# Three rearrangements in a fused attention and gated-MLP kernel: where the value means are summed, when x is copied, when the fused weights are multiplied

## The chip, the cores and the metric

The kernel runs on one core of a Trainium2 chip. The metric is the device time of one execution in microseconds (us), as the median of three runs. TensorE (PE) does matmuls and transposes into PSUM, which has eight banks of 512 fp32 columns; ScalarE (ACT), VectorE (DVE) and GpSimd (POOL) do the rest, and the SyncE queue (SP) issues all DMAs. The program is written with explicit semaphores: each engine has its own list of instructions in order, and a wait holds back everything behind it on that engine.

## The reference

Inputs are q, k, v (2 batches, 8 heads, 768 positions, 64 per head), `w_val`, `w_out` (512 x 512), 5 taps of convolution weights for 512 channels, `w_in` (512 x 1024), `w_spatial` (768 x 768), `b_spatial` and a last `w_out2`.

```
k_sum = k.reshape(B, H, nb, 32, D).max(axis=3)
v_sum = v.reshape(B, H, nb, 32, D).mean(axis=3)
scores = [q k^T / 8 where |i-j| < 16, else -1e9 ; q k_sum^T / 8 + log(32)]
x = softmax(scores) @ [v ; v_sum]                      # (B, S, 512)
gate = sigmoid(causal 5-tap convolution of x per channel)
y = (gate * (x @ w_val)) @ w_out
h = relu(y @ w_in); u, v = halves of h; v normalised over its 512 channels
out = (u * (w_spatial @ v + b)) @ w_out2
```

## The kernel before

Heads are handled in pairs: PAIRS = 8 pairs, T = 6 steps of 128 query positions for each, STEPS = 48 steps `i`, with `p, t = divmod(i, T)`. For each group of 64 queries the local keys (96) and the 24 block maxima stand side by side in `k_win` (120 columns); the local values and the 24 block means stand in `v_win`.

The loops over steps are software-pipelined by hand. In step i PE does: the scores of step i (L613), one turn (transpose) of a piece of k (t = 0, 1, 2) or q (t = 3, 4, 5) of the next pair (L578), in step 6p+2 the means of pair p (L654, six matmuls of `v_nat` with a selection matrix), the transposes of the probabilities of step i-5 (`turn_probs`, L627) and the values of step i-6 (L642). DVE masks the scores and takes their maximum (L976), normalises (L996), copies turned k (L1003) and the second head's turned q (L1014), and takes block maxima (L1029). ACT does: the copy of the turned probabilities of step i-5 (`take_probsT`, L847), in step 6p+2 the copy of the means (`take_means`, L863), the copy of the first head's turned q (L821), the exponentials of step i (L833, one for each head, each followed by a read of its accumulator), and in even steps the copies of two steps of x (L853 the first head, L856 the second; one in three of the latter is DVE's). POOL spreads the means into `v_win` (L507), then completes `k_win` of the next pair (`k_tails`, L471 to L475), splits x into two fp32r halves (L512, L526) and adds pairs of v rows ahead of the means (L495).

PSUM: banks 0 and 1 hold scores, bank 2 the turned probabilities in columns 0 to 255 and the means in 256 to 383, bank 3 reciprocals, banks 4 and 5 alternate for the turned pieces of k and q (`bank_qk(n)` is bank 4 + n % 2, columns 0 to 255, n = 0, 1, 2 for k and 3, 4, 5 for q) and later of w_out, banks 6 and 7 hold x. As the means share bank 2 with the turned probabilities, PE has ahead of the means a wait for the copy of the last probabilities, and ahead of the `turn_probs` after them one for the copy of the means (`clear_probs`).

After the steps comes a second part: 16 `val` groups (x w_val by channel block and half a batch, 12 matmuls each), 8 `fused` groups (w_out w_in, 12 matmuls each), the convolution on DVE (8 instructions for each of 8 channel blocks, L1050, after a first tap on ACT, L875, in banks 4 and 5), the gate (tanh on ACT, L887), gate times val (`work`, L1115) on DVE, its high half on ACT (L923) and low half on POOL (L526), and for fused groups a high half on ACT (L926) and a low half on DVE (L1120). The groups rotate through six banks in the order of the list `groups`: a group waits until the one six places ahead of it in the list has been taken. The lists `groups` and `between` put fused group j behind val group FUSED_AFTER[j]; ACT, DVE and POOL follow `between`. The first two val groups are computed in the last steps of attention. Then follow u, v, spatial and output groups on PE (L697 too).

## Time and profile before

| | us |
|---|---|
| median of 3 runs | 308.68 (308.52 to 309.01) |
| the profiled execution's own time | 308.57 |
| its span, first to last instruction | 306.8 |
| PE busy, PE weight loads busy | 293.8 (96%), 268.6 (88%) |
| DVE, ACT, POOL busy | 173.9, 150.9, 123.4 |

A matmul's end is modelled, so PE's busy time is not work at its peak, and a recorded end may lie behind the start of the next instruction. A wait is shown on the engine that waits, with the instruction that ended it. Times in the rows are counted from the start of the span.

### The profile page before, as it was taken

What the parts mean: (1) busy time and instruction counts of PE and PEld (TensorE: products, weight loads), DVE (VectorE), ACT (ScalarE), POOL (GpSimd) and SP (SyncE); (2) the same over time, 40 slices, a digit from 0 to 9 for tenths busy, and PEclk for the clock granted to TensorE, in tenths of its full rate; (3) what the DMA queues carried; (4) which work ended last, traced back from release to release, by engine and by line L of the source; (5) the groups of instructions that cost most, each with busy time, mean ns of one, the idle gap of its engine ahead of it and who ended that gap; (6) DMA issues with size and microseconds to landing.
All of it is one profiled execution on the core that took longest, in us unless ns stands there. A gap on an engine that the chain in (4) does not pass through costs nothing.

```text
span 306.8 us, 5354 instructions
## 1 busy us (share of the span) xinstructions
PE 293.8 (96%) x1768; PEld 268.6 (88%) x1768; DVE 173.9 (57%) x578; ACT 150.9 (49%) x464; POOL 123.4 (40%) x140
## 2 busy tenths in 40 slices
PE   7789999999999999989999999999999999999996
PEld 6788888988889899887999998888899999988885
DVE  5899888998788867778300006787755242310000
ACT  3689999999997764442422234433332111122221
POOL 6434887777534884223300001343476323220000
DMA  7999999984610633000000001121010000002222
GB/s 160 213 207 233 228 194 185 252 225 117 168 49 0 189 88 103 0 2 0 1 2 0 0 2 51 51 80 41 35 34 2 0 0 2 0 35 90 83 103 103
DMA packets 51801, 25.52 MB, mean 83 GB/s; under 512 B 44586, under 2 KB 46910, under 8 KB 51774
## 3 DMA queue, kind: packets, MB, share of 16 engines
q1 hardware_dynamic: 51774, 25.18, 33.6%
q8 instruction: 14, 0.23, 0.3%
q14 instruction: 13, 0.11, 0.1%
HBM read 22.03 MB, written 3.15 MB: 82 GB/s over the span
## 4 chain that ended last, share of the span: by engine, by line
PE 63%; ACT 20%; issue 7%; DVE 6%; POOL 2%; DMA 1%; ACTq 0%; DVEq 0%; POOLq 0%
PE psum L697 54%; ACT probs L833 7%; DVE psum L1050 4%; ACT probsT L847 2%; ACT qT L821 2%; PE psum L654 2%; ACT xT L856 2%; ACT psum L875 2%; PE psum L673 1%; PE psum L613 1%; PE psum L578 1%; ACT xT L853 1%; PE psum L785 1%; PE psum L627 1%; DVE gate L1050 1%
## 5 line engine op out<-in xcount | busy, mean ns | idle before, releaser
L526 POOL TENSOR_TENSOR g_lo<-work,g_hi 128x384 fp32r<-128x384 f32 x32 | 32.3, 1024 | 46.9 <-ACT g_hi L957 26.2
L526 POOL TENSOR_TENSOR vn_lo<-work,vn_hi 128x512 fp32r<-128x512 f32 x12 | 15.5, 1293 | 61.3 <-DVE vn_hi L1152 61.3
L833 ACT ACTIVATE probs<-neg_s,neg_max 128x120 f32<-128x120 f32 x96 | 37.0, 392 | 0.7 <-DVE neg_max L976 0.5
L642 PE MATMUL psum<-probsT,v_win 120*128 120x128 f32 x192 | 29.9, 278 | 0.0
L613 PE MATMUL psum<-k_win,qT 128*128 128x120 f32 x192 | 29.0, 274 | 0.8 <-DVE qT L1014 0.7
L976 DVE CUSTOM_DVE_ANT_0 neg_s<-psum,mask 128x120 f32<-128x120 f32 x96 | 24.6, 277 | 5.2 <-PE psum L613 4.8
L1050 DVE SCALAR_TENSOR_TENSOR psum<-xT,conv_c,psum 128x384 f32<-128x384 f32 x48 | 26.0, 616 | 1.2 <-ACT psum L875 1.0
L613 PEld LDWEIGHTS psum<-k_win,qT 128*128 128x128 f32 x192 | 25.2, 191 | 1.2 <-issue 0.9
L642 PEld LDWEIGHTS psum<-probsT,v_win 120*128 120x128 f32 x192 | 25.2, 191 | 0.8 <-issue 0.2
L1130 DVE TENSOR_TENSOR wsp_lo<-psum,wsp_hi 128x384 fp32r<-128x384 f32 x12 | 6.6, 549 | 33.3 <-ACT wsp_hi L938 33.3
L957 ACT ACTIVATE g_hi<-work 128x384 fp32r<-128x384 f32 x16 | 8.3, 523 | 34.6 <-DVE work L1164 34.6
L1162 DVE TENSOR_TENSOR work<-psum,b_row 128x384 f32<-128x384 f32 x16 | 8.9, 558 | 28.2 <-PE psum L697 26.6
L627 PE MATMUL psum<-ident,probs 128*120 128x128 f32 x96 | 19.1, 281 | 3.5 <-ACT probsT L847 3.0
L847 ACT ACTIVATE probsT<-psum 120x256 f32<-120x256 f32 x48 | 18.2, 379 | 5.1 <-PE psum L627 4.8
L931 ACT ACTIVATE u<-psum 128x384 f32<-128x384 f32 x16 | 7.9, 491 | 25.8 <-PE psum L697 25.8
L996 DVE TENSOR_TENSOR probs<-probs,psum 128x240 f32<-128x240 f32 x48 | 19.1, 400 | 1.0
L964 ACT ACTIVATE work<-psum 128x512 f32<-128x512 f32 (+1 forms) x13 | 7.3, 565 | 24.8 <-PE psum L697 23.7
L697 PE MATMUL psum<-wsp_lo,vn_hi 128*128 128x384 f32 x96 | 19.4, 336 | 0.0
L697 PE MATMUL psum<-wsp_hi,vn_lo 128*128 128x384 f32 x96 | 19.4, 336 | 0.0
L697 PE MATMUL psum<-wsp_hi,vn_hi 128*128 128x384 f32 x96 | 19.3, 335 | 0.0
L833 ACT ACTIVATION_READ_ACCUMULATOR probs<-neg_s,neg_max 128x1 f32 x96 | 18.9, 197 | 0.0
L627 PEld LDWEIGHTS psum<-ident,probs 128*120 128x120 f32 x96 | 11.1, 137 | 7.0 <-ACT probsT L847 6.2
(125 smaller groups left out, 721.1 us busy)
## 6 DMA issues: line engine op xcount, KB each, us to landing
v_win<-in_v_dram SPq DMA_DIRECT2D x16, 240.0 KB, 3.3
k_nat<-in_k_dram SPq DMA_DIRECT2D x16, 192.0 KB, 5.0
v_nat<-in_v_dram SPq DMA_DIRECT2D x8, 384.0 KB, 3.9
out_dram<-work SPq DMA_DIRECT2D x11, 256.0 KB, 2.0
q_nat<-in_q_dram SPq DMA_DIRECT2D x14, 192.0 KB, 4.4
raw<-in_moe_w_spatial_dram SPq DMA_DIRECT2D x6, 384.0 KB, 3.1
raw<-in_moe_w_out_dram SPq DMA_DIRECT2D x8, 256.0 KB, 2.8
raw<-in_moe_w_in_dram SPq DMA_DIRECT2D x8, 256.0 KB, 2.8
```

The lines of the kernel that those rows point to most:

```text
L526: nc.gpsimd.tensor_tensor(dst_lo, src, dst_hi.bitcast(F32), ALU.subtract).then_inc(lo_sem, 1)
L613: ins = nc.tensor.matmul(bank_s(i)[:, g, :], qT[:, s, 2 * t + g, :], k_win[:, s, 2 * t + g, :], start=True, stop=True)
L627: ins = nc.tensor.transpose(bank_t[:, g, :], probs[:, i % RING, g, :], ident[:, :])
L642: ins = nc.tensor.matmul(bank_x(i)[:, i % 2 * 2 + g, :], v_win[0:KEYS, s, 2 * t + g, :], probsT[0:KEYS, i % 2, g, :], start=True, stop=True)
L697: ins = nc.tensor.matmul(o, lhs[a][c], rhs[b][c], start=(part == 0 and c == 0), stop=(part == 2 and c == n - 1))
L833: ins = nc.scalar.activation(probs[:, i % RING, g, :], neg_s[:, i % 3, g, :], ACT.Exp, bias=neg_max[:, i % 4, g:g + 1], scale=-1.0, accum_ ...
L847: nc.scalar.activation(probsT[0:KEYS, i % 2, :, :], bank_t, ACT.Copy).then_inc(probsT_ready, 1)
L957: nc.scalar.activation(g_hi[:, c, w], work[:, g % 3, 0:HALF], ACT.Copy).then_inc(g2_hi_ready, 1)
L976: nc.vector.tensor_tensor_reduce(out=neg_s[:, i % 3, g, :], in0=bank_s(i)[:, g, :], in1=mask[:, e, :], scale=-(float(D) ** -0.5), scalar=B ...
L996: nc.vector.tensor_tensor(a, a, r, ALU.mult).then_inc(probs_ready, 1)
L1050: nc.vector.scalar_tensor_tensor(out=o, in0=x, scalar=w, in1=acc, op0=ALU.mult, op1=ALU.add).then_inc(conv_step, 1)
L1162: nc.vector.tensor_tensor(y, bank("spatial", g, HALF), b_row[:, w], ALU.add).then_inc(b_added, 1)
```

## The change

The means go from bank 2 to columns 256 to 383 of bank 4, and on PE from the middle of step 6p+2 to the end of steps 3, 7, 13, 19, 25, 31, 37 and 44, behind the values; ACT copies them at the beginning of the step after. The waits follow the bank: the wait for the means' copy stands ahead of `turn_k(p, 2)` from pair 2 on, of `turn_q(1, 1)` and of the later w_out turns, and no longer ahead of `turn_probs`; the means wait for the copy of the piece that was in bank 4. The second head's copy of x on ACT goes from even steps to the odd step behind. FUSED_AFTER is two larger throughout, and DVE does the next channel block's taps ahead of its part of a fused group.

```diff
--- before.py
+++ after.py
@@ -220,7 +220,7 @@
         def by_group(x):
             return x.rearrange("p (g n) -> p g n", n=GROUP)
 
-        bank_m = psum[:, 2, 2 * P:3 * P]
+        bank_m = psum[:, 4, PIECE:PIECE + P]
 
         def bank_s(i):
             return psum[:, i % 2, 0:2 * KEYS].rearrange("p (g n) -> p g n", n=KEYS)
@@ -335,6 +335,8 @@
         between += [("fused", n) for n in range(len(FUSED_AFTER), 2 * C)]
 
         LATER = 2 * (TAPS - 1)
+
+        means_at = [T // 2] + [T * p + 1 for p in range(1, PAIRS - 1)] + [STEPS - T + 2]
 
         def channels(g):
 
@@ -586,12 +588,16 @@
                     pe.wait_ge(qB_ready, PIECES * (p - 1) + 2 + piece)
                 elif piece == 2:
                     pe.wait_ge(kT_ready, PIECES * p + 1)
+                    if p >= 2:
+                        pe.wait_ge(v_mean_ready, p)
                 turn(k_nat, p, piece, k_loaded, k_turned)
 
             def turn_q(p, piece):
 
                 if piece < 2:
                     pe.wait_ge(kT_ready, PIECES * p + 2 + piece)
+                    if p == 1 and piece == 1:
+                        pe.wait_ge(v_mean_ready, 1)
                 else:
                     pe.wait_ge(qA_ready, PIECES * p + 1)
                     pe.wait_ge(qB_ready, PIECES * p + 1)
@@ -614,15 +620,10 @@
                                            start=True, stop=True)
                 ins.then_inc(scores_ready, 1)
 
-            def clear_probs(i):
-
+            def turn_probs(i):
+                pe.wait_ge(probs_ready, i + 1)
                 if i >= 1:
                     pe.wait_ge(probsT_ready, i)
-                if (i + 2) % T == 0 and i + 2 < STEPS:
-                    pe.wait_ge(v_mean_ready, (i + 2) // T + 1)
-
-            def turn_probs(i):
-                pe.wait_ge(probs_ready, i + 1)
                 for g in range(2):
                     ins = nc.tensor.transpose(bank_t[:, g, :], probs[:, i % RING, g, :], ident[:, :])
                 ins.then_inc(probs_turned, 1)
@@ -648,8 +649,11 @@
                 pe.wait_ge(v_nat_added, p + 1)
                 if p == 0:
                     pe.wait_ge(sel_step, 4)
+                    pe.wait_ge(kT_ready, 2 * PIECES)
+                elif p < PAIRS - 1:
+                    pe.wait_ge(kT_ready, PIECES * (p + 1) + 1)
                 else:
-                    pe.wait_ge(v_mean_ready, p)
+                    pe.wait_ge(wout_split, 1)
                 for j in range(RUN // 2):
                     ins = nc.tensor.matmul(bank_m[0:KEYS], sel[:, j, :], v_nat[:, p % 2, :, 2 * j * D:(2 * j + 1) * D],
                                            start=(j == 0), stop=(j == RUN // 2 - 1))
@@ -659,6 +663,7 @@
                 wait_piece(pe, W_OUT + c)
                 if c >= 2:
                     pe.wait_ge(wout_split, c - 1)
+                    pe.wait_ge(v_mean_ready, PAIRS)
                 else:
                     pe.wait_ge(qA_ready, PIECES * (PAIRS - 1) + 2 + c)
                     pe.wait_ge(qB_ready, PIECES * (PAIRS - 1) + 2 + c)
@@ -748,13 +753,11 @@
                     n, term = divmod(i - STEPS, 3)
                     val(n, (term,))
                 if 5 <= i < STEPS + 5:
-                    clear_probs(i - 5)
-                if p < PAIRS and t == 2:
-                    means(p)
-                if 5 <= i < STEPS + 5:
                     turn_probs(i - 5)
                 if 6 <= i:
                     values(i - 6)
+                if i in means_at:
+                    means(means_at.index(i))
 
             for kind, n in groups[VALS_IN:place["u", 0]]:
                 if kind == "val":
@@ -846,15 +849,18 @@
                     act.wait_ge(x_summed, i - 1)
                 nc.scalar.activation(probsT[0:KEYS, i % 2, :, :], bank_t, ACT.Copy).then_inc(probsT_ready, 1)
 
-            def take_x(j):
+            def take_xA(j):
 
                 act.wait_ge(x_summed, 2 * j + 2)
                 p, r = divmod(2 * j, T)
                 nc.scalar.activation(by_group(x_of(p, r * P, 2 * P)[0:D]), bank_x(2 * j)[0:D, :, 0:GROUP],
                                      ACT.Copy).then_inc(xA_ready, 1)
-                if not x_on_dve(j):
-                    nc.scalar.activation(by_group(x_of(p, r * P, 2 * P)[D:P]), bank_x(2 * j)[D:P, :, GROUP:P],
-                                         ACT.Copy).then_inc(xB_ready, 1)
+
+            def take_xB(j):
+
+                p, r = divmod(2 * j, T)
+                nc.scalar.activation(by_group(x_of(p, r * P, 2 * P)[D:P]), bank_x(2 * j)[D:P, :, GROUP:P],
+                                     ACT.Copy).then_inc(xB_ready, 1)
 
             def take_means(p):
                 act.wait_ge(means_summed, p + 1)
@@ -892,18 +898,20 @@
                 turned_q(0, piece)
             act.wait_ge(conv_turned, 1)
             nc.scalar.activation(conv_c[:, :], bank_x(0)[:, 0, 0:TAPS * C], ACT.Copy).then_inc(conv_ready, 1)
-            for i in range(STEPS + 7):
+            for i in range(STEPS + 8):
                 p, t = divmod(i, T)
+                if i - 1 in means_at:
+                    take_means(means_at.index(i - 1))
                 if 5 <= i < STEPS + 5:
                     take_probsT(i - 5)
-                if p < PAIRS and t == 2:
-                    take_means(p)
                 if p + 1 < PAIRS and t >= PIECES:
                     turned_q(p + 1, t - PIECES)
                 if i < STEPS:
                     exponentials(i)
                 if i >= 8 and i % 2 == 0:
-                    take_x((i - 8) // 2)
+                    take_xA((i - 8) // 2)
+                if i >= 9 and i % 2 == 1 and not x_on_dve((i - 9) // 2):
+                    take_xB((i - 9) // 2)
                 if p == PAIRS - 1 and t in WOUT_AT:
                     turned_wout(WOUT_AT.index(t))
                 if i in FIRST_AT:
@@ -1116,6 +1124,10 @@
                                                    in1=bank("val", n, HALF), op0=ALU.add,
                                                    op1=ALU.mult).then_inc(val_used, 1)
                 if kind == "fused":
+                    if n < len(FUSED_AFTER):
+                        while taps < min(LATER * (FUSED_AFTER[n] // 2 + 3), LATER * B * C):
+                            conv(taps)
+                            taps += 1
                     dve.wait_ge(fused_hi_ready, n + 1)
                     nc.vector.scalar_tensor_tensor(out=(wu_lo, wv_lo)[n // C][:, n % C, :],
                                                    in0=bank("fused", n, DM), scalar=0.5,
@@ -1166,7 +1178,7 @@
 
 RING = 6
 VALS_IN = 2
-FUSED_AFTER = (5, 7, 9, 11)
+FUSED_AFTER = (7, 9, 11, 13)
 WVALS_OF = ((), (), (0,), (1,), (2,), (3,), (), ())
 PIECES_OF = ((), (0,), (1,), (2,), (3,), (4, 5), (6,), (7,))
 WOUT_AT = (0, 1, 3, 4)
```

## Rows read from the trace of the kernel before

**Rows 1.** Busy time by stretches, one cycle of attention; columns: engine busy us, instructions, clock, DMA.
```profile
...
39.81:49.78 9.97, 9.49 (x79) 8.62 (x79) 8.89 (x47) 9.33 (x40) 7.88 (x10) 1.00 0.97 208
...
```

**Rows 2.** Waits of PE over the whole span: total us, times, longest.
```profile
...
PE psum L627 <- ACT probsT L847: 3.0, 8, 0.4
...
PE psum L697 <- DVE work L1115: 1.4, 2, 1.1
...
PE psum L697 <- ACT win_u_hi L841: 0.4, 1, 0.4
...
```

**Rows 3.** Order of time on PE in that cycle: start, us, instructions.
```profile
...
39.81 0.92 PE L654 MATMUL psum<-v_nat,sel 128*120 128x128 f32 x6
40.56 0.38 PE L627 MATMUL psum<-ident,probs 128*120 128x128 f32 x2
...
41.23 0.60 PE L613 MATMUL psum<-k_win,qT 128*128 128x120 f32 x4
...
43.81 0.43 PE L627 MATMUL psum<-ident,probs 128*120 128x128 f32 x2 [0.44 <-ACT probsT L847]
44.08 0.62 PE L642 MATMUL psum<-probsT,v_win 120*128 120x128 f32 x4
...
```

**Rows 4.** Order of time on ACT in that cycle.
```profile
...
40.98 0.38 ACT L847 ACTIVATE probsT<-psum 120x256 f32<-120x256 f32 x1 [0.47 <-PE psum L627]
41.38 0.27 ACT L863 ACTIVATE v_mean<-psum 24x128 f32<-24x128 f32 x1
41.68 0.40 ACT L833 ACTIVATE probs<-neg_s,neg_max 128x120 f32<-128x120 f32 x1
...
42.57 0.38 ACT L853 ACTIVATE xT<-psum 64x256 f32<-64x256 f32 x1
42.97 0.38 ACT L856 ACTIVATE xT<-psum 64x256 f32<-64x256 f32 x1
43.37 0.38 ACT L847 ACTIVATE probsT<-psum 120x256 f32<-120x256 f32 x1
...
45.95 0.37 ACT L853 ACTIVATE xT<-psum 64x256 f32<-64x256 f32 x1
46.22 0.38 ACT L847 ACTIVATE probsT<-psum 120x256 f32<-120x256 f32 x1
...
```

**Rows 5.** Order of time at the start, on ACT, POOL and PE.
```profile
...
12.65 0.27 ACT L863 ACTIVATE v_mean<-psum 24x128 f32<-24x128 f32 x1 [0.84 <-PE psum L654]
...
14.50 0.38 ACT L833 ACTIVATE probs<-neg_s,neg_max 128x120 f32<-128x120 f32 x1
...
12.98 1.46 POOL L507 COPY v_win<-v_mean 24x1536 f32<-24x1536 f32 x1 [1.79 <-ACT v_mean L863]
...
15.06 0.42 POOL L475 COPY k_win<-k_max 128x288 f32<-128x288 f32 x1
...
17.08 0.41 PE L578 MATMUL psum<-ident,k_nat 128*128 128x128 f32 x2 [0.75 <-ACT qT L821]
...
```

**Rows 6.** Order of time on ACT in the last pair.
```profile
...
81.34 0.39 ACT L847 ACTIVATE probsT<-psum 120x256 f32<-120x256 f32 x1
...
83.74 0.38 ACT L847 ACTIVATE probsT<-psum 120x256 f32<-120x256 f32 x1
...
```

**Rows 7.** Order of time on DVE in the second part.
```profile
...
106.77 3.24 DVE L1050 SCALAR_TENSOR_TENSOR psum<-xT,conv_c,psum 128x384 f32<-128x384 f32 x6
...
110.97 1.01 DVE L1115 SCALAR_TENSOR_TENSOR work<-gate,psum 128x384 f32<-128x384 f32 x2
115.03 0.69 DVE L1120 SCALAR_TENSOR_TENSOR wu_lo<-psum,wu_hi 128x512 fp32r<-128x512 f32 x1 [3.05 <-ACT wu_hi L926]
...
```

**Rows 8.** Order of time on PE in the second part.
```profile
...
110.94 1.10 PE L697 MATMUL psum<-win_u_hi,woutT_hi 128*128 128x512 f32 x4
...
113.74 0.86 PE L697 MATMUL psum<-x_hi,wval_hi 128*128 128x384 f32 x4
...
117.91 1.09 PE L697 MATMUL psum<-win_u_hi,woutT_hi 128*128 128x512 f32 x4
...
```

## The prediction

> **What bounds the kernel now.** I read the waits of TensorE first, then the busy time by stretches, then the order of time on each engine. The kernel has three parts: attention (0 to about 96 us, a repeating cycle of six steps for a pair of heads), the val and fused groups mixed with the convolution (about 96 to 138), and TensorE work that runs without a gap to the end. So only what moves the start of the third part moves the time. TensorE's granted clock is 1.00 (the 2.4 GHz level) in the stretch shown and plays no part.
>
> In attention the cycle is 9.97 us long: PE's weight loads fill 8.62 of it, DVE 8.89, ACT 9.33 [rows 1]. ACT is the engine to follow. It has one real gap in a cycle, 0.47 us before the copy of the turned probabilities (`take_probsT`), where it waits for PE [rows 4]. PE at that time is doing the six means matmuls (39.81 to 40.56) and only then the transposes that ACT waits for [rows 3]. This is the stall that the first part of the change is about.
>
> In the second part PE waits 0.4 us once for the high half of w_in and 1.4 us in two pieces (the longer 1.1) for DVE's `work` [rows 2]. Bank recycling is the reason: group g needs the bank of group g-6. DVE is late because it sits in order behind the copy of the fused group: it is idle 3.05 us before it [rows 7]; the next channel's taps, which need nothing of it, are queued behind.
>
> **Part 1, the means.** Call S the moment at which ACT finishes step 6p+1. Today, S to the exponentials of step 6p+2 is 1.28 us. The probabilities' copy starts at 40.98 and the first exponential at 41.68, 0.70 apart, with v_mean between them [rows 4]. The 0.47 of idle, and some 0.1 by which the last exponential before it outlasts its slot, make the rest (an estimate: 0.58).
>
> After: the means run on PE in the previous step, and that does free ACT from waiting for them. But they now lie in bank 4, and the next user of bank 4 is `turn_k(p+1, 2)`, in step 6p+2. It gets a wait for v_mean_ready, and behind it on PE's queue stands `turn_probs`, which ACT's next copy needs. ACT itself takes v_mean immediately before that copy. So ACT hands v_mean to PE and waits for PE to answer:
> - v_mean 0.27 [rows 4];
> - to PE 0.06 (the copy of 43.37 ends at 43.75, PE starts at 43.81) [rows 3, 4];
> - the two transposes of k 0.27 after a wait (43.81 to 44.08) [rows 3];
> - turn_probs 0.38 to its recorded end, and 0.04 to ACT (40.56 plus 0.38, then 40.98) [rows 3, 4].
>
> That is 1.02 us, in which ACT does only v_mean. With 0.27 for the copy (as between 45.95 and 46.22 a copy of like size [rows 4]) the exponentials start at S plus 1.29, against 1.28 today. The stall changes its name and keeps its size, in each of the six cycles with this order. I take zero. Bounds for each cycle: minus 0.2, if the hand-over is quicker for the small v_mean copy; plus 0.2, if PE's later k turn makes DVE late.
>
> The Trainium skill has the rule behind this (PSUM — Partial Sum Buffer, section PSUM bank collisions raise a hardware error): guard by bank and group of 32 partitions, not by address. By it free columns of a bank are no free bank: the wait travels with the means. The waits in the diff follow that rule; no row of before shows the new one.
>
> Two places are not regular cycles.
> - **Start.** v_mean of pair 0 is taken at 12.65 now, two steps before its new place. There it follows the exponentials of step 3, whose last starts at 14.50 [rows 5]. Without the 0.84 idle ahead of v_mean these move up a little, held by DVE's masks, so v_mean comes near 14.5, 1.85 later. POOL's spread of the means (12.98) and, in order behind it, the k tails (last one 15.06 plus 0.42) [rows 5] move by the same, to 17.3. The scores of step 6 wait for these. PE stands idle 0.75 us until 17.08 [rows 5], so that swallows most: scores to 17.85, then turn_k, 0.76 late. At the next means some 0.3 of it comes back, since they no longer stand ahead of the probabilities. Loss 0.45 (0 to 0.8); a step's exponentials and masks can take up the rest.
> - **Last pair.** From 81.34 to 83.74 ACT runs a copy, v_mean, exponentials and both x copies in 2.40 us with no gap, because the w_out copy before it covers the wait [rows 6]. After: copy 0.27, exponentials 0.75, first x copy 0.27, then S to the next copy, 1.02 plus 0.2 for the w_out turn (four transposes instead of two): 2.5. And the second x copy, 0.53 with the slower change-over, falls outside it. Together 0.55 (0.2 to 0.8) lost. PE has work ready from here on, so it reaches the end of attention.
>
> **Part 2, x in alternate steps.** The two copies take 0.40 each start to start (42.57, 42.97, 43.37), a first-head copy alone 0.27 (45.95, 46.22) [rows 4]. The sum is the same wherever the second stands, 0.81. What changes is who waits. `values` of an even step wants both halves; the second is now ready at about S plus 4.2, and PE would like to start at S plus 3.5. ACT's side: from S plus 1.29, two steps of exponentials at 0.75, three copies at 0.27 (x first head, probabilities, q) and the second x copy at 0.5. PE's side: from S plus 0.60, 26 instructions at 0.11 each (four in 0.60 less the tail of 0.17 [rows 3]), 2.9. PE loses 0.7 there, and has it to spare (8.62 of 9.97 [rows 1]); run forward at full rate, its transposes then come within 0.1 of when ACT wants them, three times in a row. I take plus 0.03 a cycle, 0.2 in all (0 to 1.2).
>
> The Trainium skill (ScalarE: Activation LUTs, Rules for kernel authors) budgets about 0.3 us an ACTIVATE plus 0.83 ns an element. For v_mean's 128 elements that is 0.41, where the row has 0.27; eight round trips would be 1.1 us dearer and the sum 309.0. The row stands.
>
> **Part 3, later fused groups and earlier taps.** PE's idle here is 1.8 us [rows 2], and since a recorded end lies 0.17 after the next start (0.92 long, next after 0.75 [rows 3]), three waits cost 2.3 in starts. The fused group two vals later asks for w_in 4.2 us later (two vals, 113.74 to 117.91 [rows 8]), so the first wait is gone. On DVE: the taps of a channel take 4.20 (106.77 to 110.97) [rows 7], two vals 0.93, a fused low half 0.61. DVE was idle 3.05 after 110.97 plus 0.93; now it goes on: taps of channel 4 to 116.1, vals 6 and 7 to 117.0, taps of channel 5 to 121.2, fused 0 to 121.84. Per channel DVE needs 5.8, PE 6.97 (110.94 to 117.91) [rows 8], so after that DVE is ahead for good. One point is tight: fused group 2 takes fused 0's bank. Fused 1 starts at 110.94 now, after two vals and fused 0 (6.97), so these started at 103.97, and without the wait of 0.44 and the 0.17 at about 103.3. From there the six vals 6 to 11 take 12.5 and fused 0 and 1 take 5.6 (2.80 each, 110.94 to 113.74 [rows 8]): PE wants the bank at 121.4 and waits 0.5. All other recycled banks are free over 1 us ahead. Net gain 2.3, less 0.5 less 0.1 for the restart: 1.7 to 2.0; I take 1.9 (0.9 to 2.4). More DVE cover (taps before fused) is free, since those taps have their first tap from ACT one gate before.
>
> **Sum.** Plus 0.45, plus 0.2, plus 0.55, minus 1.9, minus about 0.1 for v_mean standing beside an x copy: minus 0.8. The profiled execution took 308.57 with a span of 306.80; that gives 307.77 and a span of 306.0. The median of before is 0.11 above that execution: 307.9.
>
> **Rivals.**
> - *The means really leave the path.* If PE's wait is met without the round trip, each cycle wins back its 0.6, seven times: 4 us, with part 3 near 303.5 to 305. For it: the gap before the copy is real. Against: ACT's queue has v_mean directly ahead of the copy. Chance 0.08.
> - *Attention eats it all.* Round trip 0.1 dearer in eight places (an exponential is 0.38 to the next, v_mean is priced at 0.27), start and last pair at their upper bounds: 308.1 to 309.2, no change that can be told. Chance 0.30.
> - *PE becomes late in every cycle through the second x copy.* Values waits at S plus 4.2, then scores, masks and exponentials of the following steps shift; it decides from 0.25 us a cycle, when six cycles cost 1.5 more and the sum is plus 0.7: 309.4, slower; at 0.4 it is 310.3. For it: the 0.1 margins. Against: PE's 1.3 us of spare time in the cycle. Chance 0.16.
> - The forecast, 306.9 to 308.0: 0.46.
>
> **How the numbers follow.** A measurement here can tell about 0.2%, 0.6 us: below 308.06 is faster, above 309.3 slower. Faster 0.46 plus 0.08, 0.54; same 0.30; slower 0.16. The range runs from 306.5, the upper bound of part 3 with a start that loses nothing, to 309.4; it leaves out the first rival and the worse half of the third.
>
> **What the profile would show.** ACT's copy L847 still waits some 0.7 us once a cycle, with v_mean just ahead of it; PE's wait at the k turn (L578) is for v_mean; the cycle is 9.9 to 10.1 long; the waits for `work` shrink from 1.4 to about 0.5 and lie near 122; DVE never waits 3 us for wu_hi. Wrong would be: a cycle below 9.7 (the stall was not replaced) or above 10.2 (x copy), or a start of the u groups less than 1.0 earlier against the end of attention.

## The result and the profile after

The change made the kernel slower, by 0.8%: 310.96 us median (310.65 to 311.45, 4 runs) against 308.60 (308.49 to 309.01, 4 runs) for the kernel before, ratio 1.0076 [1.0058, 1.0093]. The prediction said 307.9, range 306.5 to 309.4, faster. The measured time lies above that range. The span of the profiled execution went from 306.8 to 308.9, the clock stayed at 1.00.

The first view is again the busy time of one cycle of attention (from one `v_mean` copy to the next, within 0.02 us; columns as in [rows 1]: PE, PE weight loads, DVE, ACT, POOL).
```profile
51.86:62.14 10.28, 9.03 (x78) 8.66 (x78) 9.31 (x47) 9.22 (x40) 7.87 (x9) 1.00 0.87 199
```
The cycle takes 10.28 us instead of 9.97. ACT's busy time fell, and DVE's rose from 8.89 to 9.31, but DVE has no more work to do: the durations of its 46 instructions add up to 11.9 us in a cycle of either kernel. Busy time counts overlapping records once, and they overlap less where DVE has to wait: a normalisation of 0.40 us is followed by the next mask after 0.32 where nothing waits (46.57 to 46.89 before) and after 0.42 where the mask waits (57.06 to 57.48 in the change). It is waiting that grew. PE's waits (total, times, longest), to be held against [rows 2]:
```profile
PE psum L643 <- ACT xT L862: 5.7, 8, 0.9
PE psum L580 <- ACT v_mean L869: 3.0, 6, 0.7
...
PE psum L619 <- POOL k_win L477: 1.2, 1, 1.2
PE psum L702 <- DVE wu_lo L1132: 0.9, 1, 0.9
...
PE psum L671 <- ACT v_mean L869: 0.3, 1, 0.3
```
Two of these are new in every cycle: `values` (L643) waits for the second x copy, the k turn (L580) for `v_mean`. Both stand in the order of time. PE in that cycle:
```profile
50.54 0.82 PE L658 MATMUL psum<-v_nat,sel 128*120 128x128 f32 x6
51.20 0.60 PE L619 MATMUL psum<-k_win,qT 128*128 128x120 f32 x4
52.27 0.41 PE L580 MATMUL psum<-ident,k_nat 128*128 128x128 f32 x2 [0.47 <-ACT v_mean L869]
52.52 0.38 PE L628 MATMUL psum<-ident,probs 128*120 128x128 f32 x2
...
56.32 0.68 PE L643 MATMUL psum<-probsT,v_win 120*128 120x128 f32 x4 [0.77 <-ACT xT L862]
```
and ACT:
```profile
51.45 0.38 ACT L862 ACTIVATE xT<-psum 64x256 f32<-64x256 f32 x1
51.86 0.27 ACT L869 ACTIVATE v_mean<-psum 24x128 f32<-24x128 f32 x1
52.94 0.38 ACT L850 ACTIVATE probsT<-psum 120x256 f32<-120x256 f32 x1 [0.81 <-PE psum L628]
...
55.69 0.38 ACT L862 ACTIVATE xT<-psum 64x256 f32<-64x256 f32 x1
...
57.91 0.38 ACT L850 ACTIVATE probsT<-psum 120x256 f32<-120x256 f32 x1 [0.15 <-PE psum L628]
```
The round trip is there, nearly as priced: ACT copies `v_mean` at 51.86, PE turns k at 52.27 and the probabilities at 52.52, ACT goes on at 52.94. That is 1.08 us, predicted 1.02.

**Where the time went.** The start of a step's exponentials on ACT is the common clock of both traces. After minus before: +0.72 at step 8, +0.91 at 14, +1.22, +1.58, +1.93 and +2.28 at 20, 26, 32 and 38, +2.15 at 44, +2.90 at 45, +3.45 at 46 and 47. The third val group starts 3.64 later (94.83, now 98.47), the first u group 2.11 later (149.19, now 151.30). So attention lost 3.6, and part 3 gave back 1.5.

### The profile page after: what moved, and what is told of

Same layout as the page of the kernel before. It is cut to its first block, busy times and chain, and to the rows that moved or that the text cites. A ratio compares the mean times of both kernels' runs of the same rounds, so it can differ in the third digit from the quotient of the medians.

```text
span 308.9 us, 5368 instructions
## 1 busy us (share of the span) xinstructions
PE 291.8 (94%) x1768; PEld 269.0 (87%) x1768; DVE 175.7 (57%) x578; ACT 150.7 (49%) x464; POOL 123.6 (40%) x140
## 4 chain that ended last, share of the span: by engine, by line
PE 68%; ACT 13%; issue 7%; DVE 4%; POOL 3%; DMA 2%; SPq 1%; ACTq 0%; DVEq 0%; POOLq 0%
PE psum L702 58%; ACT probs L836 8%; PE psum L643 3%; DVE psum L1058 3%; ACT xT L862 2%; PE psum L628 2%; PE psum L619 2%; DMA v_nat<-in_v_dram 2%; PE psum L580 1%; PE psum L788 1%; ACT xT L856 1%; DMA raw<-in_moe_w_in_dram 1%; DVE work L1123 1%; POOL win_u_lo L528 1%; ACT qT L824 1%
## 5 line engine op out<-in xcount | busy, mean ns | idle before, releaser
L643 PE MATMUL psum<-probsT,v_win 120*128 120x128 f32 x192 | 30.1, 279 | 5.7 <-ACT xT L862 5.7
L643 PEld LDWEIGHTS psum<-probsT,v_win 120*128 120x128 f32 x192 | 25.2, 191 | 7.7 <-issue 7.4
L628 PE MATMUL psum<-ident,probs 128*120 128x128 f32 x96 | 18.4, 273 | 0.1
L702 PEld LDWEIGHTS psum<-wsp_lo,vn_hi 128*128 128x128 f32 x96 | 17.1, 188 | 0.0
```

Source lines behind the costliest of these rows:

```text
L628: ins = nc.tensor.transpose(bank_t[:, g, :], probs[:, i % RING, g, :], ident[:, :])
L643: ins = nc.tensor.matmul(bank_x(i)[:, i % 2 * 2 + g, :], v_win[0:KEYS, s, 2 * t + g, :], probsT[0:KEYS, i % 2, g, :], start=True, stop=True)
L702: ins = nc.tensor.matmul(o, lhs[a][c], rhs[b][c], start=(part == 0 and c == 0), stop=(part == 2 and c == n - 1))
```

## The experiments

Unless said otherwise a run is after.py's code with the edit shown, in three rounds against the kernel before on the same chip. Its median was 308.72 beside the first four runs, 308.79, 308.88, 308.70 and 309.00 beside the later ones, so runs from different groups are best compared by their ratios. "Cycle" is the mean distance of two `v_mean` copies from the third to the seventh.

**1. Part 3 alone** (the kernel before with `FUSED_AFTER = (7, 9, 11, 13)` and the taps ahead of the fused copy).


> The kernel before with part 3 alone (fused groups two vals later, taps ahead of the fused low half). All theories: the second part alone wins what the changed kernel's trace shows for it. There the first u group starts 52.83 us after the third val group (98.47 to 151.30), before 54.36 (94.83 to 149.19): 1.5 us faster, 307.1. If it is under 0.5 us faster, the gain seen in the changed kernel was only attention's loss given back (DVE and ACT having had more time), and part 3 is worth little.


307.28, ratio 0.9952 [0.9937, 0.9966]; cycle 9.97. This part wins 1.4 us by itself: third val group to first u group takes 52.95, before 54.36. PE waits once:
```profile
PE psum L697 <- DVE wu_lo L1124: 1.0, 1, 1.0
```
DVE waits here as well:
```profile
106.83 0.56 DVE L1115 SCALAR_TENSOR_TENSOR work<-gate,psum 128x384 f32<-128x384 f32 x1 [1.69 <-POOL g_lo L526]
```

**2. Part 1 alone** (x copies in one step and part 3 taken back).


> The changed kernel with parts 2 and 3 undone: means in bank 4 alone. Theory X (the second x copy is what costs each cycle): cycle 9.97 to 10.05, loss only at the start (0.7) and the last pair (0.3 to 0.5): 309.6 to 310.0. Theory M (the hand-over of v_mean to PE and back costs each cycle): cycle 10.2 to 10.3, 311.0 to 311.5. Theory C (only both together cost, by PE starting late twice): like X for this run.


312.13, 1.0108 [1.0093, 1.0123]; cycle 10.27, +0.30. PE and DVE in a cycle:
```profile
51.97 0.41 PE L580 MATMUL psum<-ident,k_nat 128*128 128x128 f32 x2 [0.97 <-ACT v_mean L866]
```
```profile
52.42 0.42 DVE L1006 COPY k_win<-psum 128x256 f32<-128x256 f32 x1 [0.89 <-PE psum L580]
```
The k turn waits 0.97, and all behind it on PE with it; DVE, in order at its k copy, stands idle 0.89 (before it idles 0.42 and 0.11 in a cycle, at its masks). The hand-over on ACT, in the kernel before (which goes on as [rows 4] show) and here:
```profile
40.03 0.39 ACT L833 ACTIVATE probs<-neg_s,neg_max 128x120 f32<-128x120 f32 x1
```
```profile
51.06 0.38 ACT L836 ACTIVATE probs<-neg_s,neg_max 128x120 f32<-128x120 f32 x1
...
51.56 0.27 ACT L866 ACTIVATE v_mean<-psum 24x128 f32<-24x128 f32 x1
52.64 0.38 ACT L850 ACTIVATE probsT<-psum 120x256 f32<-120x256 f32 x1 [0.81 <-PE psum L628]
52.92 0.39 ACT L836 ACTIVATE probs<-neg_s,neg_max 128x120 f32<-128x120 f32 x1
```
From the last exponential of step 6p+1 to the first of step 6p+2 it takes 1.65 before (40.03 to 41.68) and 1.86 here (51.06 to 52.92), 0.21 more, where the prediction had 0.01. From step 6p+5 to 6p+6, 0.21 to 0.32 more are lost (1.23 to 1.34 for 1.02; the exponentials wait 0.09 for DVE's maxima there), and 0.15 comes back from step 6p+2 to 6p+3. The edit that was priced at nothing costs 0.3 a cycle with nothing else changed.

**3. Part 2 alone** (the kernel before with the x copies in alternate steps).


> The kernel before with part 2 alone: the second head's x copy on ACT a step later. Theory X: values waits for that copy as in the changed kernel (some 0.7 us, eight times) and the cycle is 10.2 to 10.3: 310.2 to 311.0. Theory M: no change, 308.4 to 308.9, cycle 9.97. Theory C: no change or under 0.4 slower, with the wait of values there but the probabilities' copy on ACT not late.


310.06, 1.0041 [1.0019, 1.0063]; cycle 10.13, +0.16. Part 2 costs too. PE:
```profile
55.15 0.68 PE L642 MATMUL psum<-probsT,v_win 120*128 120x128 f32 x4 [1.18 <-ACT xT L859]
```
The two parts are not additive: +0.30 and +0.16 alone, +0.34 together (10.31).

**4. The k turn behind the transposes of the probabilities** (all parts), so that ACT's next copy needs no answer from PE.
```
-                if p + 1 < PAIRS:
+                late = p >= 1 and t == 2
+                if p + 1 < PAIRS and not late:
                     if t < PIECES:
                         turn_k(p + 1, t)
...
                     turn_probs(i - 5)
+                if p + 1 < PAIRS and late:
+                    turn_k(p + 1, t)
```


> The changed kernel with one move: in the steps 6p+2 from pair 1 on, PE turns the third piece of k behind the transposes of the probabilities, not ahead. ACT's copy then no longer has to wait for PE to be handed v_mean. Theory M: the 0.8 us idle of ACT before that copy goes, the cycle falls from 10.32 to 9.5 or 9.6, 306.5 or less. Theory X: the idle goes too, but PE is held by the x copy at values; the cycle falls only to 9.8 to 10.0, 308.2 to 309.2. In both the start and the last pair keep their loss.


309.55, 1.0034 [1.0020, 1.0048]; cycle 10.10. ACT's 0.81 is gone, but 0.55 comes back at the copy after it:
```profile
53.51 0.38 ACT L853 ACTIVATE probsT<-psum 120x256 f32<-120x256 f32 x1 [0.55 <-PE psum L628]
```
Both cycles that had been expected (9.5 to 9.6, or 9.8 to 10.0) were missed: something else stands close behind.

**5. The same with both x copies in one step.**


> The swap of the previous kernel (third piece of k turned behind the transposes of the probabilities), and both x copies in one step again; parts 1 and 3 as changed. In the swap with alternate copies the ACT idle of 0.81 shrank to nothing but 0.55 came back one copy later, because PE, released by v_mean, needed 1.6 us to the next transposes and ACT had only 1.3 us of work. Theory chain (PE's list after the v_mean wait sets ACT's next copy): with both x copies in that step ACT has 1.8 us of work there, so the 0.55 is gone and values no longer waits for x; cycle 9.5 to 9.7, 306.3 to 307.2. Rival (DVE or PE holds the cycle, whatever ACT does): cycle stays at 9.95 or more, 308.3 or more.


309.21, 1.0011 [0.9999, 1.0024]; cycle 10.09. So with this order it makes no difference to the cycle where the second x copy stands. The theory with 9.5 to 9.7 fell, its rival (9.95 or more) stands.

**6. `v_mean` copied a step earlier**, behind the exponentials of the step in which the means run, with the second x copy behind it: all parts, and then with the order of experiment 4 as well.
```
-                if i - 1 in means_at:
-                    take_means(means_at.index(i - 1))
...
                     exponentials(i)
+                if i in means_at:
+                    take_means(means_at.index(i))
```


> The changed kernel with one move on ACT: the means' copy stands behind the exponentials of the step in which PE makes the means, ahead of the second x copy, instead of behind it. Theory chain: the x copy (0.4 us) now runs while PE answers, so ACT's idle before the probabilities' copy falls from 0.81 to 0.3 to 0.45; cycle 9.9 to 10.0, 308.6 to 309.4. Rival (the length of the cycle is set by values waiting for x): the x copy comes later, values too, and the cycle stays at 10.25 to 10.4, 310.8 to 311.3.

> Both moves, alternate x copies kept. Theory chain: cycle 9.7 to 9.9, 307.2 to 308.5; what is left is values waiting 0.7 to 0.8 for the second x copy. Rival: no better than the swap alone, cycle 10.1.


309.01, 1.0008 [0.9996, 1.0020], cycle 10.02; and 308.55, 0.9996 [0.9987, 1.0006], cycle 10.03. In neither does PE wait for `v_mean` in a regular cycle, and `values` still waits 0.77 for the second x copy. The second kernel had been expected at 9.7 to 9.9. The early copy with both x copies in one step was not tried.

**7. The start** (experiment 5's kernel, `means(0)` a step earlier).


> As the kernel with the swap and the x copies together, but the means of pair 0 at the end of step 2 instead of 3. If the start's loss (0.7 us in the changed kernel) comes from POOL's spread and k tails behind the late v_mean, PE's 1.2 us wait for k_win goes and the time is 0.4 to 0.8 below that kernel; if it comes from the load of k of pair 2, it stays.


310.03, 1.0040 [1.0020, 1.0059], against 309.21 in experiment 5. The profiled execution was the fastest of the six (309.28), its span is 307.6, 0.2 below that of experiment 5 (307.8), and the traces of the two run level from step 14 on (at step 38 +0.67 and +0.69 against before); so the traces don't show what makes the median 0.8 higher. PE's wait for the k window's tails is gone, and nothing lasting comes of it: the 0.24 won at step 8 is down to 0.03 at step 14.

**8. DVE's chain** (experiment 5's kernel; in step 6p+2 DVE takes `max_k(p + 1, 1)` and the next `normalise` ahead of the k copy it waits for).


> The kernel with the swap and both x copies in one step, and one move on DVE: in steps 6p+2 the block maxima of the second piece and the next normalisation stand ahead of the copy of the third piece of k, behind which DVE idled 0.90 us a cycle, waiting for PE, which waited for v_mean. Theory DVE chain (in that kernel the cycle of 10.09 is 0.90 of idle and 9.19 of unbroken DVE work): some 0.7 us of work fills the idle, cycle 9.4 to 9.6, five cycles and a half, 305.8 to 306.8. Rival (another loop of PE and ACT is as long, as in the before kernel at 9.97): cycle 9.9 to 10.05, 308.2 to 309.


309.35, 1.0016 [1.0003, 1.0029]; cycle 10.07. The theory that the idle DVE sets the cycle fell: filled at one place, the idle time came up at the next. But the rows showed who holds whom. PE:
```profile
52.34 0.41 PE L580 MATMUL psum<-ident,k_nat 128*128 128x128 f32 x2 [0.64 <-ACT v_mean L869]
52.58 0.67 PE L643 MATMUL psum<-probsT,v_win 120*128 120x128 f32 x4
53.09 0.60 PE L619 MATMUL psum<-k_win,qT 128*128 128x120 f32 x4
```
DVE:
```profile
52.78 0.42 DVE L1009 COPY k_win<-psum 128x256 f32<-128x256 f32 x1 [0.26 <-PE psum L580]
53.73 0.28 DVE L982 CUSTOM_DVE_ANT_0 neg_s<-psum,mask 128x120 f32<-128x120 f32 x1 [0.52 <-PE psum L619]
```
ACT:
```profile
51.92 0.27 ACT L869 ACTIVATE v_mean<-psum 24x128 f32<-24x128 f32 x1
59.27 0.39 ACT L839 ACTIVATE probs<-neg_s,neg_max 128x120 f32<-128x120 f32 x1 [0.26 <-DVE neg_max L982]
```
That is a closed loop: `v_mean`, k turn, values and, behind them in PE's order, the scores of step 6p+3; DVE's masks; DVE without a gap above 0.04 us until 59.27; exponentials that wait for it; the next `v_mean`.

**9. The last pair's means back** in the old bank, step and order, with all parts; then in experiment 8's kernel; then in the second kernel of 6.
```
+        def bank_m(p):
+            return psum[:, 2, 2 * P:3 * P] if p == PAIRS - 1 else psum[:, 4, PIECE:PIECE + P]
```


> The changed kernel, with the means of the last pair alone in their old bank, step and order. From the exponentials of step 38 to those of step 47 the changed kernel needs 1.17 us more than before, and means alone 0.7, x alone 0.4. Theory: the last pair's hand-over of v_mean ahead of the w_out turn is the 0.7: 310.0 to 310.4. Rival (ACT's own list is the length there, as no copy waits before): no change, 310.8 to 311.1.

> The DVE move and the last pair's old order together. If both theories hold, the effects add: 0.6 to 1.2 below the kernel with the DVE move, 304.9 to 306.0, below the kernel with part 3 alone (307.3).

> Changed kernel with early means' copy, swap and the last pair's old order, x copies in alternate steps. Cycle stays at 10.03 as with both moves; the last pair gives back 0.7 to 1.2: 307.3 to 307.9. If the last pair's loss was ACT's own list, 308.4 to 308.7.


310.08, 1.0049 [1.0034, 1.0064]; 308.49, 0.9989 [0.9979, 0.9999]; 308.37, 0.9986 [0.9976, 0.9995]. From step 38 to 47 the first loses 0.32 where the change loses 1.17. The second is 0.9 us below experiment 8's kernel in the median, the third 0.2 below its own (0.3 by the ratios); in the traces both lose 0.6 less from step 38 to 47. The totals that had been expected for these two (304.9 to 306.0, 307.3 to 307.9) were missed.

**10. The k turn behind the scores** (parts 1 and 3, x copies in one step). The loop of experiment 8 is cut where it closes.
```
                     scores(i)
-                if p + 1 < PAIRS:
+                late = p >= 1 and t == 2
+                if p + 1 < PAIRS and p >= 1 and t == 3:
+                    turn_k(p + 1, 2)
+                if p + 1 < PAIRS and not late:
...
+                    if t == 3 and p >= 1:
+                        turned_k(p + 1, 2)
                     if t < PIECES:
-                        turned_k(p + 1, t)
+                        if t != 2 or p == 0:
+                            turned_k(p + 1, t)
```
The second place is DVE's list, behind the masks of step 6p+3.


> Parts 1 and 3, both x copies in one step; in the regular cycles the third k piece's transposes now stand behind the scores of step 6p+3, and DVE's copy of that piece behind that step's masks. So the one thing that waits for v_mean has neither the transposes of the probabilities nor any scores behind it for a whole step. Theory A, that TensorE's in-order wait for v_mean, through the scores and masks behind it, holds the cycle at 10.0 to 10.1 us in all variants so far: cycle 9.5 to 9.8, five cycles give back 1 to 2.5 us, total 306.8 to 308.3. Theory B, that the cycle is bound by ACT and DVE taking turns (their own work, whoever waits for v_mean): cycle 9.95 to 10.1, total 308.8 to 309.4. Theory C, that the k turn a step later makes the k maximum and so normalise or the next masks late: cycle above 10.2, total above 309.8.


305.24, 0.9888 [0.9873, 0.9903]; cycle 9.36 to 9.52, mean 9.42, better than any of the theories had it. One cycle of it, then ACT, then PE:
```profile
50.00:59.36 9.36, 9.20 (x79) 8.48 (x78) 8.95 (x47) 9.20 (x40) 7.89 (x10) 1.00 1.04 219
```
```profile
50.00 0.27 ACT L869 ACTIVATE v_mean<-psum 24x128 f32<-24x128 f32 x1
50.29 0.38 ACT L853 ACTIVATE probsT<-psum 120x256 f32<-120x256 f32 x1
50.57 0.39 ACT L839 ACTIVATE probs<-neg_s,neg_max 128x120 f32<-128x120 f32 x1
```
```profile
50.12 0.60 PE L619 MATMUL psum<-k_win,qT 128*128 128x120 f32 x4
50.56 0.38 PE L580 MATMUL psum<-ident,k_nat 128*128 128x128 f32 x2
```
ACT is busy for 9.20 of 9.36 us and waits for nobody. The k turn starts at 50.56, after `v_mean` ended at 50.27.

**11. The same with the last pair's means back.**


> The run before it, and the last pair's means back in the old bank, step and order. By the earlier pair of runs this takes 0.9 us off whatever the cycle is: A 306.0 to 307.4, B 307.9 to 308.5, C above 308.9. If below 307.2 it would be the fastest version and the freed bank would be of use after all.


305.05, 0.9878 [0.9859, 0.9898]. The last pair's hand-over, in the kernel of 10 and then in this one, on ACT:
```profile
80.89 0.27 ACT L869 ACTIVATE v_mean<-psum 24x128 f32<-24x128 f32 x1
82.19 0.38 ACT L853 ACTIVATE probsT<-psum 120x256 f32<-120x256 f32 x1 [1.03 <-PE psum L628]
```
```profile
79.89 0.38 ACT L857 ACTIVATE probsT<-psum 120x256 f32<-120x256 f32 x1
80.30 0.27 ACT L873 ACTIVATE v_mean<-psum 24x128 f32<-24x128 f32 x1
```
Step 44 to 45 costs 1.15 less, but step 38 to 44 costs 0.60 more, as `v_mean` then stands ahead of the exponentials of step 44 again. From step 38 to 47 the gain is 0.60, as in the two pairs of experiment 9. The medians are 0.2 apart and their intervals overlap; the profiled execution began 0.6 later than that of experiment 10. So the gain is seen in the trace, not in the total.

**12. No means in the cycles** (experiment 1's kernel; block means of the first pair only, used for all; this leaves out part of the computation).


> The kernel before with part 3 alone, but the block means are computed for the first pair only and used for all (the outputs of pairs 1 to 7 are not the reference's): no means matmuls, no v_mean copy and no wait for it in the cycles. This is the most that any place for the means can give. Theory A (the 0.47 us stall and the 0.27 us copy are on the path): cycle 9.2 to 9.4, total 302.5 to 304. Theory B (another loop, DVE and ACT taking turns, stands close behind): cycle 9.8 to 9.95, total 306.2 to 307.2. Between: the share of the stall that was ever to be had.


301.57, 0.9774 [0.9759, 0.9790]. There is but one `v_mean`, so the exponentials are the clock: against before they gain 3.35 us from step 14 to 38, four cycles, 0.84 each (9.13; 9.2 to 9.4 had been expected). This is what the means cost in all. The kernel of 10 wins 0.55 a cycle by the same count (2.19 in four), and its `v_mean` copy (50.00 to 50.29) is 0.29. The two add up to the 0.84: by this count nothing is left over.

**13. Control: the k turn late, means in the old place** (experiment 1's kernel with the edit of 10).


> Control: the kernel before with part 3, the means in their old bank, step and order, and only the third k piece's transposes and its copy moved one step later. Theory A (the means had to leave ACT's path and the wait for them TensorE's): ACT still waits 0.47 us for the transposes behind the means matmuls, cycle 9.8 to 10.0, total 306.5 to 307.6. Theory B (the gain comes from the k turn's new place alone, the means' bank is beside the point): cycle 9.4 to 9.6, total 304.5 to 306.


307.34, 0.9950 [0.9936, 0.9964]; cycle 9.97, and the old gap is as it was:
```profile
51.20 0.38 ACT L850 ACTIVATE probsT<-psum 120x256 f32<-120x256 f32 x1 [0.47 <-PE psum L627]
```
The gain of 10 needs part 1 and the new place for the k turn; the place alone gives nothing. Part 1 moves the means to another bank and to an earlier step on PE; these two were not tried apart.

**14. The whole change with the k turn late**, x copies in alternate steps.


> The whole change as made, with the one edit of the run that brought the cycle to 9.42: the third k piece's transposes behind the scores of step 6p+3 and DVE's copy of it behind that step's masks. Theory A (the 0.31 us a cycle that the change cost was TensorE held at v_mean with the scores behind it; x in alternate steps costs little once that loop is gone): cycle 9.4 to 9.55, total 305.0 to 306.3. Theory B (the second x copy makes values late by itself, 0.1 to 0.2 a cycle as in the run of part 2 alone): cycle 9.55 to 9.8, total 306.3 to 307.8.


308.61, 0.9982 [0.9969, 0.9994]; cycle 9.89. PE, then ACT:
```profile
54.94 0.68 PE L643 MATMUL psum<-probsT,v_win 120*128 120x128 f32 x4 [0.77 <-ACT xT L865]
```
```profile
52.88 0.38 ACT L853 ACTIVATE probsT<-psum 120x256 f32<-120x256 f32 x1 [0.34 <-PE psum L628]
...
56.53 0.38 ACT L853 ACTIVATE probsT<-psum 120x256 f32<-120x256 f32 x1 [0.15 <-PE psum L628]
```
The alternate copies cost 0.47 a cycle as soon as nothing else holds it: PE waits 0.77 in `values`, and ACT gets 0.34 and 0.15 of it back as waits for the transposes behind. Both theories fell: I had expected that x would be nearly free (cycle 9.4 to 9.55), or cost 0.1 to 0.2 as in experiment 3 (9.55 to 9.8).

**15. The k turn late in the first pair's steps too**, on the kernel of 11.


> The version with the k turn a step later and the last pair's means in their old place, with the k turn a step later for the first pair's cycle too (10.1 us there, 9.4 in the others). If the same wait holds that cycle: 0.3 to 0.6 less, total 304.4 to 304.8. If it is held by the start (the k window's tails from POOL): no change, 305.0; if the later k turn makes k maximum and the following scores late there: 305.3 to 305.8.


305.51, 0.9891 [0.9864, 0.9919]: no gain to be told. It was also aimed badly. The long cycle (10.1) runs from step 8 to 14 and had the late k turn already; this edit touches steps 2 and 3. Of the 0.7 by which that one cycle is longer, the trace of experiment 10 shows 0.6 as waits that the later cycles don't have, 0.34 at 21.71 for PE's transposes and 0.26 at 28.48 for DVE's maxima, both on ACT:
```profile
21.71 0.38 ACT L853 ACTIVATE probsT<-psum 120x256 f32<-120x256 f32 x1 [0.34 <-PE psum L628]
...
28.48 0.40 ACT L839 ACTIVATE probs<-neg_s,neg_max 128x120 f32<-128x120 f32 x1 [0.26 <-DVE neg_max L982]
```
PE comes to the first of them without a gap since its wait for the k window's tails (until 17.45), so the late start is a likely cause; that wasn't tried on this kernel.

## Why the prediction was wrong

The cycles in one table (us; mean of the steady ones):

| | x copies in one step | in alternate steps |
|---|---|---|
| k turn ahead of turn_probs, as changed | 10.27 | 10.31 |
| behind turn_probs, ahead of the scores | 10.09 | 10.10 |
| behind the scores of step 6p+3 | 9.42 | 9.89 |
| means in the old place | 9.97 | 10.13 |

- **Part 1, zero a cycle: the step that failed.** The hand-over was found, and the wait sits where it was said: L580, for `v_mean`, six times. Trainium skill, PSUM — Partial Sum Buffer, section PSUM bank collisions raise a hardware error: the wait travelled with the bank, as the rule has it. But the balance that gave zero, 1.28 against 1.29 from S to the next exponentials, failed twice. On ACT itself it measured 0.21 and not 0.01 (experiment 2): the round trip took 1.08 for 1.02, and `v_mean` starts 0.50 after the last exponential, where the next instruction mostly starts after 0.38, which the sum had left out. And the balance was struck for ACT alone. The prediction itself gave a bound of plus 0.2 "if PE's later k turn makes DVE late", and took zero. Before, PE does the six means while ACT waits, then goes on; now PE has done the means early and stands idle for the same hand-over, with turn_probs, values and the scores of step 6p+3 behind it, and DVE idles 0.89 behind that (experiment 2). Cost alone: +0.30. Experiments 10 and 13 show that the k turn's place in PE's queue decides, once part 1 is in.
- **What it took to see the rest.** Two loops stood at nearly the same length: the wait for `v_mean` with the scores behind it (10.09 with x in one step) and the late second x copy (9.89 with the first out of the way, 10.02 and 10.03 in experiment 6, where PE waits for that copy and not for `v_mean`; why it is 0.13 more there stays open). Taking away one shows little, since the other is close behind: experiments 4 to 8 all ended between 10.02 and 10.10. Both are gone only with the late k turn and x in one step.
- **Part 2, plus 0.03 a cycle: wrong too,** the second failed step. "PE loses 0.7 there, and has it to spare" is half right: PE waits 0.77 in the change, 1.18 alone. But spare time in an average cycle isn't spare at that place, as the transposes for ACT's next two copies stand directly behind `values`. +0.16 alone, +0.47 with the loop of part 1 cut. This is the third rival's mechanism; its threshold of 0.25 a cycle was passed (0.34), though by both parts together. The cycle passed the 10.2 that the prediction had named as a sign of being wrong; it had put that down to the x copy, but of the 0.34 part 1 makes 0.30 alone.
- **Start, 0.45.** The k tails ran where forecast:
```profile
14.90 1.46 POOL L509 COPY v_win<-v_mean 24x1536 f32<-24x1536 f32 x1 [3.49 <-ACT v_mean L869]
...
16.97 0.42 POOL L477 COPY k_win<-k_max 128x288 f32<-128x288 f32 x1
17.45 0.70 PE L619 MATMUL psum<-k_win,qT 128*128 128x120 f32 x4 [1.18 <-POOL k_win L477]
```
  With the order of experiment 4 step 8 is 0.27 late, in the change 0.72: the other 0.45 is the first hand-over. Experiment 7 took PE's wait away and won nothing lasting.
- **Last pair, 0.55: too small.** Its own terms (2.5 for 2.40, and 0.53 for the second x copy) add up to 0.63. The hand-over was priced at 1.22 there (1.02 and the w_out turn), and took 1.30:
```profile
85.34 0.27 ACT L869 ACTIVATE v_mean<-psum 24x128 f32<-24x128 f32 x1
86.64 0.38 ACT L850 ACTIVATE probsT<-psum 120x256 f32<-120x256 f32 x1 [1.03 <-PE psum L628]
```
  Step 44 to 45 lost 0.75 and the next step, which got the second x copy, 0.55 more: 1.30 in all, counted from the exponentials of step 44, ahead of which `v_mean` no longer stands. Counted from copy to copy, as the prediction did, it is 2.71 for 2.40 (83.93 to 86.64) and the 0.55: 0.86. Old means in that place save 0.85 (experiment 9).
- **Part 3, minus 1.9: the mechanism was right, the size was not.** It measured 1.53 in the change and 1.41 alone. PE's one wait is the one foreseen, for the bank of fused 0, 0.9 instead of 0.5. DVE was later than worked out. `work` has three buffers, and at the pair of vals ahead of the taps DVE waits for POOL's `g_lo`:
```profile
110.17 0.55 DVE L1123 SCALAR_TENSOR_TENSOR work<-gate,psum 128x384 f32<-128x384 f32 x1 [1.63 <-POOL g_lo L528]
...
125.31 0.68 DVE L1132 SCALAR_TENSOR_TENSOR wu_lo<-psum,wu_hi 128x512 fp32r<-128x512 f32 x1
```
  That wait was 1.35 before, at 106.30, and lay hidden in the 106.77 from which the prediction counted [rows 7]; it grew to 1.69 in experiment 1, where `wu_lo` starts at 121.97 and not at 121.2. Of these 0.8 us, 0.2 are the later end of attention, 0.3 that wait, the rest small change.
- **The sum.** Measured: 0.27 start; 1.88 from step 8 to step 44, with the first hand-over; 1.30 last pair; 0.19 from there to the third val group; minus 1.53: +2.11, the shift of the first u group. Predicted: 0.45, 0.2, 0.55, minus 1.9, minus 0.1. Of the 2.9 us between, 2.4 are the cycles and the last pair together (counted from copy to copy, 2.1 the cycles and 0.3 the last pair), 0.4 part 3, and the rest is small. The terms that the prediction names for the lower end of its range give 306.95 and not 306.5 (0.5 and 0.45 less than 307.9); this has no bearing on the miss.
- **The price of `v_mean`.** The 0.41 us that the prediction works out for `v_mean` from the Trainium skill (ScalarE: Activation LUTs, Rules for kernel authors) is, by the same line there, for an ACTIVATE whose bias is a pointer operand. The copy of the means has none, and takes 0.27 all eight times in both kernels; the row was the right price.
- **The first rival** ("the means really leave the path", each cycle 0.6 less) was not what this diff does, but what it lacked one edit for: 0.55 a cycle. ACT's queue, held against it, was not what decided; PE's was.

The fastest versions that compute everything are those of experiments 10 and 11: 305.24 and 305.05, 1.1 to 1.2% below the kernel before. They keep parts 1 and 3, undo part 2 and turn the third k piece behind the scores of the next step; the second also takes the last pair's means back.

## What to carry to other kernels

When a wait moves to another engine's queue, strike the balance for that engine and for what stands behind the waiting instruction there (here the scores, so DVE's masks), not only for the engine that the move relieves. If an edit that takes away a visible wait changes nothing, a second loop of nearly the same length may stand behind it: try the two together, and run a version that leaves the disputed work out, since it tells how much there is to win. A new home for data in a bank is worth its price only if the bank's next user is placed late enough to find it free.

## What the runs showed of the hardware

- An ACT copy of x's second head costs more than its own time. In the change the exponentials before it give way after 0.50 (50.95 to 51.45), where two exponentials lie 0.38 apart, and the next instruction starts 0.41 after it (51.86); a first-head copy hands on after 0.28 (53.98 to 54.26). Both kinds of row say 0.36 to 0.38 busy. It is so at all 11 second-head copies between 20 and 80 us. The copy of the means is like it: 0.50 behind an exponential (51.06 to 51.56 in experiment 2) and 0.40 behind a copy (40.98 to 41.38 before). The second head's output starts at partition 64, that of the means at 96, but before, 6 of 18 first-head copies too start 0.50 after an exponential (42.07 to 42.57), so the partition isn't the whole cause; it wasn't tried. The Trainium skill (ScalarE: Activation LUTs, What ACT_TABLE_LOAD costs) lets back-to-back ACTIVATEs overlap by about 93 ns: the first-head rows agree (0.36 busy, 0.28 start to start), the second-head rows don't (0.38 busy, 0.41).
- The time from an ACT copy's end to a PE matmul that waits for it, 0.14 in the cycle (52.13 to 52.27), is more than the 0.06 that the prediction took from [rows 3, 4]; the same step reads 0.15 in experiment 8 (52.19 to 52.34).
